# Attention and two feed-forward layers on one core: the up-projections by seven products in place of eight

## The reference

```python
scores = q @ k.T / sqrt(64); keep keys that are sinks (first 4) or 0 <= query - key < 128
x = softmax(scores) @ v                      # 2 batches, 8 heads, 768 tokens, head size 64
x = x laid out as [1536 tokens, 512]
h = x @ w_in;  g = h * clip(h + 3, 0, 6) / 6;        x = g @ w_out      # w_in [512, 2048], w_out [2048, 512]
h = x @ w2_in; g = h * (1 / (1 + exp(-1.702 * h)));  y = g @ w2_out     # the same sizes
```

## Time and profile before

| | |
|---|---|
| median of 3 runs | 631.14 us (630.48 to 632.81) |
| the profiled execution | 632.29 us, its span 630.5 us |
| TensorE busy | 614.2 us, 97% of the span |
| VectorE, ScalarE, GpSimd busy | 234.7, 222.6, 154.3 us |
| matmuls | 3328, of them 2304 in the feed-forward layers |
| moved by DMA | 29.81 MB |

### The profile page before, as it was taken

One profiled execution on the slowest core, in us unless ns is written; L12 is line 12 of the kernel. 1 busy time (PEld: TensorE's weight loads), 2 busy tenths in 40 slices (PEclk: granted clock), 3 DMA queues, 4 the chain that ended last, 5 costly groups with the idle time before them and its releaser, 6 DMA issues.

```text
span 630.5 us, 9468 instructions
## 1 busy us (share of the span) xinstructions
PE 614.2 (97%) x3328; PEld 510.8 (81%) x3328; DVE 234.7 (37%) x557; ACT 222.6 (35%) x474; POOL 154.3 (24%) x131
## 2 busy tenths in 40 slices
PE   5999988999999999999999999999999999999997
PEld 4888877888888888888888888888888888888885
DVE  4778774222233222233333642222432224322222
ACT  5777773444332222232222332222322223222121
POOL 7778830544300000004666560000000000000000
PEclk9999998999999999999999999999999999999999
DMA  6245101322300000000223110000010000100001
GB/s 235 79 161 186 58 26 68 107 95 99 101 1 1 0 2 1 0 0 34 99 100 100 68 66 0 1 1 0 1 68 1 0 1 0 67 0 0 0 0 67
DMA packets 9227, 29.81 MB, mean 47 GB/s; under 512 B 1072, under 2 KB 1392, under 8 KB 9200
## 3 DMA queue, kind: packets, MB, share of 16 engines
q1 hardware_dynamic: 9200, 29.46, 13.8%
HBM read 26.31 MB, written 3.15 MB: 47 GB/s over the span
## 4 chain that ended last, share of the span: by engine, by line
PE 95%; DVE 1%; issue 1%; DMA 1%; ACT 1%; POOL 0%; SPq 0%; DVEq 0%; ACTq 0%; POOLq 0%
PE psum L785 14%; PE psum L787 14%; PE psum L786 14%; PE psum L815 7%; PE psum L813 7%; PE psum L817 7%; PE psum L814 7%; PE psum L818 7%; PE psum L819 7%; PE psum L764 4%; PE psum L721 3%; PE psum L734 3%; PE psum L768 1%; DMA raw<-qk 1%; PE psum L749 1%
## 5 line engine op out<-in xcount | busy, mean ns | idle before, releaser
L785 PE MATMUL psum<-x_split,weights 128*128 128x512 f32 x384 | 149.6, 390 | 0.0
L787 PE MATMUL psum<-x_split,weights 128*128 128x512 f32 x384 | 149.4, 389 | 0.0
L786 PE MATMUL psum<-x_split,weights 128*128 128x512 f32 x384 | 149.4, 389 | 0.0
L679 DVE TENSOR_TENSOR gated_split<-gated,gated_split 128x512 fp32r<-128x512 f32 x96 | 74.9, 781 | 182.3 <-ACT gated_split L547 182.3
L547 ACT ACTIVATE gated_split<-gated 128x512 fp32r<-128x512 f32 x96 | 60.7, 632 | 192.3 <-PE psum L819 96.1
L785 PEld LDWEIGHTS psum<-x_split,weights 128*128 128x128 f32 x384 | 72.0, 188 | 15.2 <-issue 0.3
L787 PEld LDWEIGHTS psum<-x_split,weights 128*128 128x128 f32 x384 | 72.1, 188 | 15.0
L786 PEld LDWEIGHTS psum<-x_split,weights 128*128 128x128 f32 x384 | 72.1, 188 | 15.0
L446 POOL TENSOR_TENSOR weights<-stage,weights 128x1024 f32 x28 | 70.7, 2525 | 43.5 <-ACT weights L552 40.6
L817 PE MATMUL psum<-weights,gated_split 128*128 128x512 f32 x192 | 74.8, 390 | 0.8 <-DVE gated_split L679 0.8
L818 PE MATMUL psum<-weights,gated_split 128*128 128x512 f32 x192 | 74.7, 389 | 0.0
(11 more groups left out here) (63 smaller groups left out, 661.7 us busy)
## 6 DMA issues: line engine op xcount, KB each, us to landing
stage<-w SPq DMA_DIRECT2D x32, 512.0 KB, 3.3
raw<-qk SPq DMA_DIRECT2D x7, 776.0 KB, 5.1
values<-v_keys SPq DMA_DIRECT2D x8, 384.0 KB
out<-y_stage SPq DMA_DIRECT2D x12, 256.0 KB, 2.1
raw<-qk SPq DMA_DIRECT2D x1, 264.0 KB, 2.8
raw<-qk SPq DMA_DIRECT2D x2, 128.0 KB, 2.1
raw<-qk SPq DMA_DIRECT2D x1, 256.0 KB, 3.6
sink_values<-v_sinks SPq DMA_DIRECT2D x8, 4.0 KB
```

What stands on the lines that cost most here:

```text
L679: dve.tensor_tensor(gated_split[:, f % 2, 1, :], gated[:, f % 2, :], gated_split[:, f % 2, 0, :].bitcast(F32), ALU.subtract).then_inc(g_re ...
L785: pe.matmul(h, w_high_d, x_split[:, 0, d, :], start=d == 0, stop=False)
L786: pe.matmul(h, w_high_d, x_split[:, 1, d, :], start=False, stop=False)
L787: last = pe.matmul(h, w_low_d, x_split[:, 0, d, :], start=False, stop=d == DB - 1)
```

## The change

The up-projection of a pair of hidden blocks (block p and block p + 8, so that the pair is a 2 x 2 arrangement of quarters: 256 inner features by 128 hidden ones, against 256 tokens) is computed by Strassen's scheme in the form with seven products, each 2 inner blocks x 3 matmuls of 256 columns. The seven products lie in four PSUM banks. Four of the seven weight operands and four of the seven token operands are sums or differences. `combine` on VectorE adds the products in four instructions into a `hidden` tile in SBUF, after a copy of the first product by ScalarE; the gates then read SBUF in place of PSUM. `down` keeps its matmuls, for two blocks at a time. TensorE's order is up(p), down(p - 1).

The up-weights no longer stay in SBUF: SP loads them for each pair of each chunk, GpSimd makes the four sums and all low parts, ScalarE the high parts, into a ring of two. The down-weights are still split once per layer, in the layer's first chunk, by ScalarE and VectorE. The token operands of the next chunk are renewed one by one as the PSUM banks of the last pair's products are done (`DONE_IN_BANK`), their sums in pairs 3 to 6. In the last attention body `during` puts in the first two pairs' weights on GpSimd and the first token sums and splits on VectorE and ScalarE; TensorE's drain is written out anew with the first up in three pieces. ScalarE, VectorE, GpSimd and SP have their feed-forward parts written out step by step in place of loops.

```diff
+        DONE_IN_BANK = [1, 2, 2, 3, 3, 4, 4]
+        SUM_OF_X = {2: (0, 3), 3: (1, 1), 4: (2, 2), 6: (3, 4)}
...
+            for p in range(2):
+                load_up(0, p)
+                load_down(0, p)
             load_body(HEAD_PAIRS - 1)
...
+            for layer, c in CHUNKS:
+                for p in range(PAIRS):
+                    n = (layer * NCHUNK + c) * PAIRS + p
+                    if n >= 2:
+                        sp.wait_ge(up_ready, 4 * (n - 1))
+                        load_up(layer, p)
+                        if c == 0:
+                            sp.wait_ge(down_ready, layer * PAIRS + p - 1)
+                            load_down(layer, p)
...
-            pipelined(pool, [once_a_group(D_LAG, widen), (0, split_next_pair), (0, early_weights)], peel_last=True)
...
+            def up_sums_first(n):
+                raw_n = up_raw[:, n % 2, :, :]
+                pool.wait_ge(up_loaded[n % 2], 16 * (n // 2) + 16)
+                if n:
+                    pool.wait_ge(up_ready, 4 * n)
+                pool.tensor_tensor(up_sums[:, 1, :], raw_n[:, 2, :], raw_n[:, 3, :], ALU.add).then_inc(up_summed, 1)
+                pool.tensor_tensor(up_sums[:, 2, :], raw_n[:, 0, :], raw_n[:, 2, :], ALU.subtract).then_inc(up_summed, 1)
+
+            def up_sums_second(n):
+                raw_n = up_raw[:, n % 2, :, :]
+                pool.wait_ge(up_summed, 4 * n + 1)
+                pool.tensor_tensor(up_sums[:, 0, :], up_sums[:, 1, :], raw_n[:, 0, :], ALU.subtract).then_inc(up_summed, 1)
+                pool.wait_ge(up_summed, 4 * n + 3)
+                pool.tensor_tensor(up_sums[:, 3, :], raw_n[:, 1, :], up_sums[:, 0, :], ALU.subtract).then_inc(up_summed, 1)
+
+            def up_low(n, part):
+                at, source, needed = ((slice(0, 2), up_raw[:, n % 2, 0:2, :], 1), (slice(6, 7), up_raw[:, n % 2, 3:4, :], 2),
+                                      (slice(2, 4), up_sums[:, 0:2, :], 3), (slice(4, 6), up_sums[:, 2:4, :], 3))[part]
+                pool.wait_ge(up_rounded, 3 * n + needed)
+                pool.tensor_tensor(up_split[:, n % 2, 1, at, :], source, up_split[:, n % 2, 0, at, :].bitcast(F32),
+                                   ALU.subtract).then_inc(up_ready, 1)
+
+            def up_high(n):
+                pool.tensor_copy(up_split[:, n % 2, 0, 0:2, :], up_raw[:, n % 2, 0:2, :]).then_inc(up_rounded, 1)
+                pool.tensor_copy(up_split[:, n % 2, 0, 6, :], up_raw[:, n % 2, 3, :]).then_inc(up_rounded, 1)
+                pool.wait_ge(up_summed, 4 * n + 4)
+                pool.tensor_copy(up_split[:, n % 2, 0, 2:6, :], up_sums[:, :, :]).then_inc(up_rounded, 1)
+
+            def first_weights(s):
+                if s == 1:
+                    up_sums_first(0)
+                if s == 2:
+                    up_sums_second(0)
+                if s == 3:
+                    up_high(0)
+                if s == 5:
+                    up_low(0, 0)
+                    up_low(0, 1)
+                if s == 6:
+                    up_low(0, 2)
+                if s == 7:
+                    up_low(0, 3)
+                if s == 8:
+                    up_sums_first(1)
+                if s == 9:
+                    up_sums_second(1)
+                if s == 10:
+                    up_high(1)
+
+            def second_weights(s):
+                if s == 0:
+                    up_low(1, 0)
+                    up_low(1, 1)
+                if s == 1:
+                    up_low(1, 2)
+                    up_low(1, 3)
...
+            up_sums_first(2)
+            up_sums_second(2)
+            for n in range(2, STEPS):
+                for part in range(4):
+                    up_low(n, part)
+                if n + 1 < STEPS:
+                    up_sums_first(n + 1)
+                    up_sums_second(n + 1)
...
+            def round_x(chunk, q):
+                x_valid(act, chunk)
+                if q in SUM_OF_X:
+                    act.wait_ge(x_summed, 4 * chunk + SUM_OF_X[q][1])
+                if chunk:
+                    act.wait_ge(products_ready, 4 * (chunk * PAIRS - 1) + DONE_IN_BANK[q])
+                act.activation(x_split[:, 0, q, :, :], x_operand(chunk % NCHUNK, q), ACT.Copy).then_inc(x_hi_ready, 1)
+
+            def round_up_raw(n):
+                act.wait_ge(up_loaded[n % 2], 16 * (n // 2) + 16)
+                if n >= 2:
+                    act.wait_ge(products_ready, 4 * (n - 1))
+                act.activation(up_split[:, n % 2, 0, 0:2, :], up_raw[:, n % 2, 0:2, :], ACT.Copy).then_inc(up_rounded, 1)
+                act.activation(up_split[:, n % 2, 0, 6, :], up_raw[:, n % 2, 3, :], ACT.Copy).then_inc(up_rounded, 1)
+
+            def round_up_sums(n):
+                act.wait_ge(up_summed, 4 * n + 4)
+                act.activation(up_split[:, n % 2, 0, 2:6, :], up_sums[:, :, :], ACT.Copy).then_inc(up_rounded, 1)
+
+            def first_splits(s):
+                if s == 9:
+                    round_x(0, 0)
+                if s == 11:
+                    for q in range(1, 4):
+                        round_x(0, q)
+
+            def last_splits(s):
+                if s == 1:
+                    round_x(0, 4)
+                    round_x(0, 5)
+                if s == 3:
+                    round_x(0, 6)
...
+                    if n and n + 1 < STEPS:
+                        round_up_raw(n + 1)
+                        round_up_sums(n + 1)
+                    if c == 0:
+                        round_down(layer, p)
+                    if p == 1 and chunk:
+                        empty(chunk - 1)
+                    copy_first(n)
+                    if new_x:
+                        for q in range(5):
+                            round_x(chunk + 1, q)
+                    gate(layer, n, 0)
+                    if new_x:
+                        round_x(chunk + 1, 5)
+                    gate(layer, n, 1)
+                    if new_x:
+                        round_x(chunk + 1, 6)
+                    round_product(n, 0)
+                    round_product(n, 1)
...
+            def first_splits(s):
+                if s == 9:
+                    sum_x(0, 0)
+                    sum_x(0, 1)
+                if s == 11:
+                    sum_x(0, 2)
+                    sum_x(0, 3)
+                    low_x(0, 0)
+
+            def last_splits(s):
+                if s == 1:
+                    for q in range(1, 4):
+                        low_x(0, q)
+                if s == 3:
+                    for q in range(4, PRODUCTS):
+                        low_x(0, q)
...
+            def combine(n, new_low=lambda q: None):
+                new_low(0)
+                dve.wait_ge(first_copied, n + 1)
+                dve.wait_ge(products_ready, 4 * n + 2)
+                dve.tensor_tensor(hidden[:, :, :].rearrange("p (a b) t -> p a b t", a=2)[:, :, 0, :], in_bank(1),
+                                  hidden[:, 7:8, :].to_broadcast([P, 2, HALF_CHUNK]), ALU.add).then_inc(combined, 1)
+                new_low(1)
+                dve.wait_ge(combined, 4 * n + 1)
+                dve.wait_ge(products_ready, 4 * n + 3)
+                dve.tensor_tensor(hidden[:, 5:7, :], in_bank(2), hidden[:, 4:5, :].to_broadcast([P, 2, HALF_CHUNK]), ALU.add
+                                  ).then_inc(combined, 1)
+                new_low(2)
+                dve.wait_ge(combined, 4 * n + 2)
+                dve.tensor_tensor(hidden[:, 3, :], product_at(3), hidden[:, 6, :], ALU.add).then_inc(combined, 1)
+                dve.wait_ge(products_ready, 4 * n + 4)
+                dve.tensor_tensor(hidden[:, 1:3, :], in_bank(3), hidden[:, 5:7, :], ALU.add).then_inc(combined, 1)
+                new_low(3)
...
+                    if new_x:
+                        combine(n, lambda q: low_x(chunk + 1, q))
+                    else:
+                        combine(n)
+                    gate(layer, n, 0)
+                    if new_x:
+                        low_x(chunk + 1, 4)
+                    gate(layer, n, 1)
+                    if new_x:
+                        low_x(chunk + 1, 5)
+                    low_product(n, 0)
+                    if new_x:
+                        low_x(chunk + 1, 6)
+                    low_product(n, 1)
+                    if more and 3 <= p < 7:
+                        sum_x(chunk + 1, p - 3)
...
+            def up(chunk, p, qs=range(PRODUCTS)):
+                n = chunk * PAIRS + p
+                for q in qs:
+                    if q == 0:
+                        pe.wait_ge(up_ready, 4 * n + 4)
+                    if p == 0:
+                        pe.wait_ge(x_ready, PRODUCTS * chunk + q + 1)
+                    if due(n):
+                        if q == 0:
+                            pe.wait_ge(first_copied, n)
+                        elif q % 2:
+                            pe.wait_ge(combined, 4 * n + (-3, -1, 0)[q // 2])
+                    for d in range(2):
```

(27 more changed lines are left out.)

439 lines of the change are left out of this document (202 added, 237 removed).

## The result

The changed kernel took 622.92 us (median of 4 runs, 621.64 to 625.09), the kernel before 631.19 (4 runs): a ratio of 0.987, 95% interval 0.983 to 0.991. Two repeats, on other chips, gave 0.990 (0.988 to 0.992) and 0.989 (0.987 to 0.991). The forecast was 617 us with 603 to 633 around it: the direction is right, the gain is 8 us in place of 14. The profiled execution's span went from 630.5 to 623.3, so 7.2 us are to be accounted for.

The account below looks back on a forecast made before the run. TensorE's matmul stream was taken as the bound. Terms of -21.2, +3, +6.5, -1.4 and -0.8 sum to -13.9 us, taking the profiled 632.3 to 618.4, or 617 us as the median; range 603 to 633.

Parts of the forecast that it names:

- Part 1: Up-projection: 42 matmuls of 256 columns per pair, 0.119 us apart, in place of 24 long ones; -21.2 us.
- Rival C: Up-projection: short matmuls start 0.11 us apart, giving 599 us; chance 0.05.
- rival D: Up-projection: short matmuls start 0.13 us apart or more, giving 639 us; chance 0.05.
- Part 2: Steady pair: helper engines, even with GpSimd and VectorE colliding, fit within TensorE's 10.44 us, so TensorE sets the pace.
- Parts 3 and 4: Chunks making down-weights and token operands renewed at chunk ends: TensorE stalls of +3 and +6.5 us.
- part 3: Chunks making down-weights: a serial ScalarE-VectorE chain of 10.6 to 11 us per pair exceeds TensorE's 10.44; +3 us.
- rival B: Feed-forward stream: the port shared with VectorE makes GpSimd the bound, giving 638 us (631 to 645); chance 0.12.
- Part 5: Last attention body and drain: the feed-forward stream starts earlier despite added helper work; -1.4 us (-5 to +4).
- TensorE wants them at 81.39: +1.4: Last attention body: GpSimd is ready for the last pair's scores only at about 82.8 us, costing 1.4 us.
- Three new VectorE instructions (2.0 us): Drain: VectorE's new instructions ahead of the normalisation take 2.0 us, leaving TensorE 2.6 us idle.
- The tail: End of the kernel: the 0.83 us wait for the last low part goes; -0.8 us.
- A: Feed-forward stream: all helper work hides, no stalls in down-weight chunks or at chunk ends; 608 us; chance 0.22.

Follow-up runs that it names:

- short_256: The kernel before with every 512-column up matmul split into two of 256, nothing else; 647.4 us, ratio 1.026 to the kernel before.
- down_late2: down_late with SP asking for the next up-weights first and, in the last pair, the seventh token low part ahead of the down-weights' one; 621.1 us, ratio 0.985.
- low_memset: The changed kernel with GpSimd's low parts of the up-weights replaced by memsets to zero, which read nothing; 612.7 us, ratio 0.971 to the kernel before.
- body_late: The changed kernel with GpSimd's first weight sums and casts moved from steps 1 to 3 of the last attention body to step 5 and later; 622.0 us, ratio 0.986.
- down_late: The changed kernel with down-weights rounded behind the first product's copy, their low part behind the pair's low products (last pair: ahead); 631.5 us, ratio 1.001.
- drain_mid: The changed kernel with three of VectorE's token low parts later in the drain, one behind the first normalisation, two behind the second; 623.3 us, ratio 0.988.
- pool_late: The changed kernel with GpSimd's work for the second weight pair put behind its last attention work; 623.6 us, ratio 0.989 to the kernel before.
- drain_late: The changed kernel with VectorE's last two token sums and first low part moved behind the drain's normalisation and copies; 625.8 us, ratio 0.993.
- best_b: best_a with drain_mid's order on VectorE as well; 620.6 us.
- best_a: The changed kernel with down_late2 and body_late together; 620.1 us, ratio 0.983 to the kernel before.
- after_third: The changed kernel itself, unaltered, run again as a yardstick beside the variants; 624.3 or 624.4 us, as its two repeats gave.

## Why the prediction was right, and where it was off

**Part 1, the products: right.** 0.119 was put, 0.120 measured; -21.2 became -19.2. short_256 shows the 0.120 without the seven products. Rival C, at 0.11, is refuted by it, rival D's 0.13 too.

**Part 2, the steady pair: right.** 10.44 was put, 10.50 measured in chunks 1, 2, 4 and 5, and no start there is over 0.06 us late. VectorE's instructions with two SBUF inputs took 923 and 939 ns on average in place of 690, and GpSimd still paused 1.5 us per pair, as the prediction's signs had it.

**Parts 3 and 4: the sum right (9.5 put, 8.4 measured), the chain right, its working not.** The terms that part 3 lists for the chain add up to 10.35 us, which is under TensorE's 10.44 and would make no stall; the text says 10.6 to 11. It leaves out ScalarE's copy of the first product (0.4), and with it they make 10.75. The measured chain is 10.74: the +3 came out well partly by luck. The chain does set the rounds of chunk 0's first half, and down_late2, which takes the down-weights out of it, has rounds of 10.50. But TensorE doesn't wait at the gated low parts there, as was put: it waits at the head of each up for GpSimd's low parts of the up-weights, which hang on the same chain (some 0.2 us at each, 0.7 at one). In the chunk's second half GpSimd has hardly a pause left, rival B's mechanism, confined to these pairs. low_memset shows that both need the lengthening or GpSimd's own time: with VectorE's instructions at their own length and GpSimd's short, no start is late. By place: inside chunk 0 1.8 us (+3 put), at its end 4.3 (+5), at the end of chunk 3 2.2 (+1), elsewhere nothing (+0.5). The 4.3 are 2.1 us of waits for x_split, 0.9 for up-weights, and up to 0.26 more with each of the five, 0.16 at the start itself and 0.10 at the next one.

**Part 5: wrong, and this is the miss.** -1.4 was put, +4.1 measured. The steps cost more than that, 5.3 us: this execution came to the last body 1.2 us earlier than the one before (scores at 69.40 against 70.60), and that is chance, as traces with the same code up to there lie up to 1.6 us apart. Its steps:
- "TensorE wants them at 81.39: +1.4": from the pair before, the scores came 2.0 us late; body_late takes the wait away. The sum for GpSimd had no pause in it, but ahead of one widening it waited 1.22 us for VectorE's denominators (71.4 to 72.7).
- The clock was left out. Behind the 1.7 us wait the eight transposes at 83.78 took 1.92 us, 1.11 before, and the next scores came 5.37 us later in place of 3.91: +1.5. This one belongs to the execution and not to the kernel alone: of nine traces with this same wait six show the lower clock behind it, while in down_late, down_late2 and drain_mid it stayed at 1.00 and the transposes took 1.11. Behind the 4.0 us wait the transposes and first value products ended at 104.2, 4.5 us after the restart; 2.8 was put, though before the change the first up also began 4.5 us behind its restart at 96.11, at 100.59 (line below).
- "Three new VectorE instructions (2.0 us)": they took 3.6, since GpSimd's second weight pair runs beside them. pool_late shows them at 2.1 and the wait at 2.4, close to the 2.6 that the forecast had. The prediction had weighed the lock in the stream and left it out in the drain, where it placed GpSimd's work itself.
- The two sums in step 9 took 1.8 and put TensorE off by 1.15, where 0.6 was put.

The line of the kernel before:

```profile
100.59 0.50 PE L785 MATMUL psum<-x_split,weights 128*128 128x512 f32 x1
```

The tail is as put. Of the rivals, A (all hides) misses the 8.4 us, and B's time, 631 or more, didn't come. The total lies in the range by no cancelling of large errors: +2.0 in part 1, -1.1 in parts 3 and 4, +5.5 in part 5.

What stays open: how the 8.4 us part between the lock and GpSimd's length, what makes the 0.120 of a short matmul, and whether the drain has an order that saves its 5 us of waits: drain_late only moved them, drain_mid saved 1.5 us in its trace but not clearly in the time, and best_b gained nothing on best_a.

## What to carry to other kernels

An algorithm with fewer products pays per matmul: count what a short one costs beyond its columns (here 0.013 us on 0.107), and measure it by splitting the old matmuls. Work given to idle engines is charged with the instructions it lengthens: for each helper with two SBUF inputs, list what GpSimd reads at the same moment, in the start-up too. When a step moves later in an engine's order, look at what waits for it and at what it now stands ahead of: down_late made SP's queue late, but lost its 7 us by the 1.2 us low part that it put ahead of the last token one. Add up a chain's terms again, and count the pauses of a helper that itself waits.

## What the runs showed of the hardware beyond what was expected

- Float32r matmuls with a load of 128x128 weights each start 0.2267 us apart at 512 columns and 0.120 at 256 (short_256 and the changed kernel), 0.013 us above 512 and 256 columns at 2.4 GHz; transposes of 128 columns with such a load start 0.119 apart. Whether the 0.120 is columns and a fixed part or the time of a load isn't shown.
- A wait of 1.7 us in the last attention body, behind a stretch of short transposes and value products, was followed by work at the lower clock in six traces of nine (1.92 us for eight transposes, 1.11 at the full one), with the same code up to there.
- Behind the waits of 0.2 to 0.9 us at the end of chunk 0 the granted clock stayed at 1.00 in the changed kernel's first trace, and was 0.50 from 193.8 to 197.2 us in after_third's.
- A wait in the stream cost 0.23 to 0.26 us more than the idle time shown, spread over its own start (0.16) and the next.
